# Two buffers for a batch's attention rows, and its sums of squares moved into the units of the next batch

## What is computed

```python
# 1. gated linear attention: B,H,S,D = 4, 8, 768, 48
for t in range(S):
    state = alpha[:, :, t, :, None] * state + np.einsum('bhd,bhe->bhde', k[:, :, t], v[:, :, t])
    y[:, :, t] = np.einsum('bhd,bhde->bhe', q[:, :, t], state)
x = attn_out.transpose(0, 2, 1, 3).reshape(B * S, H * D)      # 3072 rows of 384
# 2. mixture of 8 experts, one for each row, 384 -> 1024 -> 384
xn = x / (np.linalg.norm(x, axis=-1, keepdims=True) + 1e-06)  # needs a sum of squares of each row
logits = xn @ en.T / tau;  expert_idx = np.argmax(logits, axis=1)
out[mask] = gate_w[mask, None] * (np.maximum(x[mask] @ w1[e], 0.0) @ w2[e])
# 3. h = max(x @ w1, x @ w2, x @ w3), then h @ w_out, 384 -> 768 -> 384
```

## Time and profile before

| | |
|---|---|
| median of 3 runs | 801.3 us (801.27, 801.3, 805.0) |
| the profiled execution, its own time | 803.54 us |
| its span, first to last instruction | 801.8 us |
| TensorE busy (matmuls) | 749.3 us, 93% of the span |
| VectorE, GpSimd, ScalarE busy | 378.7, 296.7, 274.1 us |
| mean granted TensorE clock | 0.975 of full |

### The profile page before, as it was taken

How to read it: one execution, slowest core, us unless ns; L and a number is a source line. 1 busy time by engine, 2 the same in 40 slices (tenths; PEclk the granted TensorE clock), 3 DMA queues, 4 the chain that set the end, 5 groups by cost and what they waited for, 6 DMA issues and landing times.

```text
span 801.8 us, 15838 instructions
## 1 busy us (share of the span) xinstructions
PE 749.3 (93%) x4774; PEld 659.5 (82%) x4775; DVE 378.7 (47%) x708; ACT 274.1 (34%) x638; POOL 296.7 (37%) x226
## 2 busy tenths in 40 slices
PE   3998989989299999999999999999999999999995
PEld 3887878878269999999999888888888888888885
DVE  6787877856763343424243327533333333333321
ACT  6677776774322232222222222211211111111110
POOL 3243334410146457536275498513123131220011
PEclk9999999989689999999999999999999999999999
DMA  9966475530648154443333202101101011000001
GB/s 182 272 121 153 91 169 107 100 89 2 220 164 330 38 190 146 165 141 108 128 108 118 90 22 61 31 20 40 30 30 41 20 39 30 20 20 0 11 20 49
DMA packets 128789, 74.48 MB, mean 93 GB/s; under 512 B 103448, under 2 KB 122016, under 8 KB 128736
## 3 DMA queue, kind: packets, MB, share of 16 engines
q1 hardware_dynamic: 118624, 53.53, 24.9%
q0 software_dynamic: 4096, 10.24, 3.4%
q10 hardware_dynamic: 6016, 10.07, 3.4%
HBM read 59.03 MB, written 14.79 MB: 92 GB/s over the span
## 4 chain that ended last, share of the span: by engine, by line
PE 78%; issue 13%; DVE 3%; POOL 2%; ACT 2%; DMA 0%; ACTq 0%; POOLq 0%; DVEq 0%
PE bank L1421 55%; PE bank L1220 4%; PE bank L1313 3%; PE bank L1457 3%; PE bank L1250 3%; PE bank L1302 3%; PE bank L1281 2%; PE bank L1294 1%; PE bank L1268 1%; PE bank L1407 1%; POOL out L530 1%; DVE Sm L891 1%; PE bank L1479 1%; ACT sq L653 1%; DVE low1h L1041 1%
## 5 line engine op out<-in xcount | busy, mean ns | idle before, releaser
L490 POOL TENSOR_TENSOR wsp<-raw,wsp 128x1536 f32 x28 | 103.8, 3725 | 91.7 <-DVE wsp L1106 91.7
L1421 PE MATMUL bank<-yh,mh 128*128 128x512 f32 x324 | 128.1, 396 | 0.0
L1421 PE MATMUL bank<-yh,ml 128*128 128x512 f32 x324 | 126.5, 390 | 0.0
L530 POOL DMA_INDIRECT out<-oo,tok_t x24 | 24.2, 1010 | 199.9 <-DVE oo L1163 199.9
L1421 PE MATMUL bank<-yl,mh 128*128 128x512 f32 x324 | 91.4, 390 | 0.0
L1421 PE MATMUL bank<-wsp,xh 128*128 (+1 forms) x324 | 85.3, 398 | 3.8 <-issue 3.2
L1421 PE MATMUL bank<-wsp,hTh 128*128 x432 | 81.8, 340 | 0.0
L809 ACT CAST gh<-t 128x512 fp32r<-128x512 f32 x36 | 22.3, 620 | 151.5 <-DVE t L1174 151.5
L1421 PEld LDWEIGHTS bank<-wsp,hTh 128*128 128x128 f32 x432 | 73.9, 188 | 0.2 <-issue 0.2
L1421 PEld LDWEIGHTS bank<-wsp,xh 128*128 128x128 f32 x324 | 58.9, 188 | 15.9 <-issue 4.1
L1421 PEld LDWEIGHTS bank<-yl,mh 128*128 128x128 f32 x324 | 60.8, 188 | 13.0
(11 more groups left out here) (205 smaller groups left out, 1321.2 us busy)
## 6 DMA issues: line engine op xcount, KB each, us to landing
raw<-in_moe_w SPq DMA_DIRECT2D x16, 1536.0 KB, 7.8
expert_rows<-ye ACTq DMA_DIRECT2D x27, 193.0 KB, 3.5
yg<-expert_rows SPq DMA_DIRECT2D x24, 193.0 KB, 2.5
nat<-in_alpha SPq DMA_DIRECT2D x32, 144.0 KB, 2.7
nat<-in_k SPq DMA_DIRECT2D x32, 144.0 KB, 2.9
nat<-in_q SPq DMA_DIRECT2D x32, 144.0 KB, 3.0
vt<-in_v SPq DMA_DIRECT2D x32, 144.0 KB, 3.0
attention_rows<-xc SPq DMA_DIRECT2D x4, 1152.0 KB, 5.1
```

The source lines that it names most:

```text
L490: g.tensor_tensor(wsp[:, ds(to, 1), 1, n, part], raw[:, n:n + 1, part], wsp[:, ds(to, 1), 0, n, part].bitcast(f32), ALU.subtract).then_inc ...
L530: g.indirect_dma_start(out=out, out_offset=bass.IndirectOffsetOnAxis(ap=tok_t[:, i, 0:1], axis=0), in_=oo[i % 2][:], in_offset=None).then_ ...
L1421: last = mm(o, x, y, start=(n == 0), stop=(n == len(todo) - 1))
```

## The change

There are now two buffers `xc`, used in turn by the batches. `squares` does one chunk at a call. Of batch b-1's six, two stand in each of the units j = 0, 1, 2 of batch b: one behind `check_a`, ahead of `carry(u, 1)`, and one behind `stage_x`, ahead of the next unit's `stage_c`. The last batch's six still stand at the end. The wait for the store of rows now is for the one two batches earlier. The buffer `junk` is gone, which makes room for the second `xc`: `check_a` writes its unused copy into `kpT` (units 0 and 1) or into the `aT` whose scans are done, and `stage_a` has a wait more for that. ScalarE's and SyncE's loops over the batches are written out; those of PE, VectorE and GpSimd stay.

```diff
-    xc = sb("xc", [P, CH, DM])
+    xc = [sb(f"xc{i}", [P, CH, DM]) for i in range(2)]
-    junk = sb("junk", [P, S])
...
-            sp.dma_start(xv[:, ds(b, 1)], xc[:].rearrange("p (o c) n -> p o c n", o=1)).then_inc(x_out, 16)
+            sp.dma_start(xv[:, ds(b, 1)], xc[b % 2][:].rearrange("p (o c) n -> p o c n", o=1)).then_inc(x_out, 16)
...
-        with sp.Fori(0, B - 1) as b:
+        for b in range(B - 1):
...
             act.wait_ge(dve_A, CR + u - 1)
+            if u >= 4:
+                act.wait_ge(act_sumA, CR + u - 1)
...
         def check_a(u, j):
             act.wait_ge(act_sumA, CR + u)
-            a.activation(junk[:], A[j][:], ACT.Copy, accum_out=sums[:, 0, ds(u, 1)]).then_inc(act_sumA, 1)
+            left = (kpT[:].rearrange("p c n -> p (c n)") if u < 2 else aT[u % 2][:])
+            a.activation(left, A[j][:], ACT.Copy, accum_out=sums[:, 0, ds(u, 1)]).then_inc(act_sumA, 1)
...
         def stage_x(b, u, j):
-            if j == 0:
-
-                act.wait_ge(x_out, CR + 16 * b)
+            if j == 0 and b >= 2:
+
+                act.wait_ge(x_out, CR + 16 * (b - 1))
...
-        def squares(b):
+        def squares(b, c):
             act.wait_ge(act_X, CR + 8 * b + 8)
-            for c in range(CH):
-                act.wait_ge(act_ss, CR + CH * b + c)
-                a.activation(sq[:], xc[:, c, :], ACT.Square, accum_out=ss[:, ds(CH * b + c, 1)]).then_inc(act_ss, 1)
-
-        def step(b, j, base):
+            act.wait_ge(act_ss, CR + CH * b + c)
+            a.activation(sq[:], xc[b % 2][:, c, :], ACT.Square,
+                         accum_out=ss[:, CH * b + c:CH * b + c + 1]).then_inc(act_ss, 1)
+
+        def step(b, j):
             u = UPB * b + j
-            if j:
+            if u:
                 stage_c(u)
-            if base + j + 2 < NU:
+            if u + 2 < NU:
                 stage_a2(u + 2, (j + 2) % UPB)
             carry(u, j, 0)
-            if base + j + 2 < NU:
+            if u + 2 < NU:
                 check_a(u + 2, (j + 2) % UPB)
+            if b and j < CH // 2:
+                squares(b - 1, 2 * j)
             for c in range(1, CH - 1):
                 carry(u, j, c)
             stage_y(b, u, j)
-            if base + j + 3 < NU:
+            if u + 3 < NU:
                 stage_a(u + 3, (j + 3) % UPB)
             stage_x(b, u, j)
+            if b and j < CH // 2:
+                squares(b - 1, 2 * j + 1)
...
+        act.wait_ge(act_sumA, CR + 2)
         stage_c(0)
-        with act.Fori(0, B - 1) as b:
+        for b in range(B):
             for j in range(UPB):
-                step(b, j, 0)
-            stage_c(UPB * b + UPB)
-            squares(b)
-        for j in range(UPB):
-            step(B - 1, j, NU - UPB)
-        squares(B - 1)
+                step(b, j)
+        for c in range(CH):
+            squares(B - 1, c)
```

More of the change, by code:

```diff
@@ L204, in build @@
     assert cur[0] <= ff_low
-    router_const = (top - 4096) // 512 * 512
+    router_const = (top - 3072) // 512 * 512
     cur[0] = router_const
@@ L347, in _ @@
                 sp.wait_ge(s_done, CR + UPB * b + UPB)
-                sp.dma_start(xv[:, ds(b, 1)], xc[:].rearrange("p (o c) n -> p o c n", o=1)).then_inc(s_out, 16)
+                sp.dma_start(xv[:, ds(b, 1)], xc[0][:].rearrange("p (o c) n -> p o c n", o=1)).then_inc(s_out, 16)
         sp.wait_ge(r_hot, 1)
@@ L633, in stage_x @@
                 got = bank[6 + h][:, 0:HC * (P + E)].rearrange("p (c n) -> p c n", c=HC)
-                rows = xc[:, HC * h:HC * h + HC, HD * j:HD * j + HD]
-                a.copy(lgp[:, ds(CH * b + HC * h, HC), j, :], got[:, :, P:P + E])
+                rows = xc[b % 2][:, HC * h:HC * h + HC, HD * j:HD * j + HD]
+                a.copy(lgp[:, CH * b + HC * h:CH * b + HC * h + HC, j, :], got[:, :, P:P + E])
                 a.copy(rows.rearrange("p c (h d) -> p c h d", h=2),
@@ L642, in place @@
                 got = bank[2 + h][:, 0:HC * (P + E)].rearrange("p (c n) -> p c n", c=HC)
-                rows = xc[:, HC * h:HC * h + HC, HD * j:HD * j + HD]
+                rows = xc[0][:, HC * h:HC * h + HC, HD * j:HD * j + HD]
                 a.copy(lgp[:, ds(CH * b + HC * h, HC), j, :], got[:, :, P:P + E])
@@ L719, in _ @@
                             act.wait_ge(s_pl if c == 0 else s_sq, b + 1 if c == 0 else CR + CH * b + c)
-                            a.activation(sq[:], xc[:, c, :], ACT.Square,
+                            a.activation(sq[:], xc[0][:, c, :], ACT.Square,
                                          accum_out=ss[:, ds(CH * b + c, 1)]).then_inc(s_sq, 1)
```

## The result

The changed kernel took 790.06 us in the median of four runs (788.71 to 790.78), the one before 801.28 us in four runs beside it (800.96 to 805.0). The ratio is 0.9846, 95% interval 0.9823 to 0.987: faster by 1.5%, 11.2 us. The prediction was 786.8 us, range 784.8 to 791.0.

A forecast was written before the change was run, and what follows sets the result against it. TensorE was taken to set the attention stage's pace, waiting at batch ends for ScalarE's late states. -10.1 - 4.6 + 0.1 = -14.6, rounded to -14.5: 803.54 to 789.0, less 2.24 gives 786.8 us; range 784.8 to 791.0.

The forecast's parts named there:

- the three units: Attention units 4, 8 and 12 at the batch ends: 15.23, 15.35 and 15.96 us against 10.63 for an ordinary unit.
- The excess of 14.65 us: Time of units 4, 8 and 12 beyond 10.63 us each, all of it predicted to go.
- lateness: At batch ends, carried states come late because ScalarE does six squares first: 10.1 us, predicted to go.
- the clock: TensorE's granted clock drops to 0.50 after its idle time at batch ends: 4.6 us, predicted to go.
- The higher price of 0.74: Upper bound in us for one square, from the loop's spacing, which includes a wait for the square before.
- Unit 15: Unit 14's second square delays unit 15's `kpT`, with 0.45 us spare: costs 0.1 us, at most 0.3.
- the 2.24 us: Other runs' median lies this far below the profiled 803.54 us; subtracted from 789.0 to give 786.8 us.
- the first (squares show in part): Rival: first square delays the carries by at most 0.18 us in nine units, 1.6 us back, 788.4; chance 9%.
- the fourth (ScalarE the bound): Rival: both squares fall on the path in nine units, each gap lowering TensorE's clock: 811.6 us; chance 2%.
- first place: Between `check_a` and `carry(u, 1)` on ScalarE: cover of 1.10 us against a square's 0.52 to 0.74, costs nothing.
- The second (the clock stays low): Rival: low clock at batch ends has another cause or residual idle suffices; 4.6 us stay, 791.4; chance 4%.
- The third (the wait changes its name): Rival: something else at batch ends is late by 3.5 us or more each time, 797.3 or above; chance 3%.

The follow-up runs named there:

- the block: Changed kernel with all six squares of a batch in one block behind the next unit's kpT, where they stood before: 802.11 us, ratio 1.0009 to the kernel before.
- the second profile: The changed kernel run and profiled again with no edit: median 789.28 us, profiled execution 788.88 us.
- the third profile: The kernel before, profiled a third time with no edit: one run, 800.61 us.
- the kernel that keeps TensorE at work: Kernel before with three discarded products added ahead of TensorE's UA wait in units 4, 8 and 12, its loop written out: 798.07 us, ratio 0.9942.

## Why the prediction was right, and where it was off

- **What bounds the stage, and why the three units are long**: right. The beats are 10.63 us with the squares spread and 14.87, 13.37 and 14.90 us again with the block.
- **The excess of 14.65 us goes**: right in size, 14.55 us in the profile. Of its parts, lateness was taken too large and the clock too small: 10.1 and 4.6 us; with the clock held up the lateness is 9.0, so the clock had 5.65 in that execution. The sum counted the slow clock only in the eighteen instructions behind the carried states. Part of what it called lateness was slow clock already: at the first end the sixteen products from 74.09 us on took 1.58 us and at the third those from 168.25 on 1.97, against 1.31 at 121.19.
- **The eighteen squares cost nothing, at 0.52 us each**: right, 0.09 us after a read, the idle time for `V` nearly used up, no delay. The higher price of 0.74 would have been hidden too: with one more square there, 0.63 + 0.52 us, only 0.12 us leak through in every second unit.
- **Unit 15, 0.1 us, at most 0.3**: TensorE's wait is 0.28 us, and the last two units together are 0.35 us longer. The ceiling, not the value.
- **Second buffer, written-out code, added waits: nothing**: right, ratio 1.0009 (0.9991 to 1.0026) for these alone.
- **The time of the profiled execution, 789.0 us**: it was 790.78, and 788.88 in the second profile.
- **The step that failed** is the one ahead of the number: "The median of the other runs is 2.24 us lower, 801.3, so I predict 786.8 us". I took the 2.24 us as something that both kernels share. To a large part they are the removed part itself. The excess of the three units is 14.65 us in the profiled execution, of 803.54 us, but 11.8 us in the third profile, of 800.61 us: the low clock lasts 13.6 us there in the one and 6.8 in the other. An execution that has less of it can win only less. From 801.9 us, the median over 42 runs, to 789.5 over eight it is 12.4 us, between 11.8 and 14.65. The clock's part, 5.65 us in the profiled execution, is 801.9 - 798.07 = 3.8 us between medians, by the kernel that keeps TensorE at work (5.5 us against the eleven runs beside it, more of which were of the upper group). With it, 9.0 + 3.8 - 0.1 - 0.35 = 12.4 us, which fits.
- **What is left of the miss**: 786.8 is 3.3 us below the 790.06 measured. This step is 2.2 of them. In the other 1.0 are unit 14's square, 0.35 us where 0.1 was counted, and the collision at the start of the third layer, 1.7 us in the profiled execution; how many of the timed runs have it is not known.
- **The range held in part by luck**: the time lies in its upper part, which was kept for the first two rivals, and neither of them is what filled it.
- **Rivals**: the first (squares show in part) and the fourth (ScalarE the bound) did not happen. With two squares more in each first place TensorE does wait for ScalarE, but then it is 0.6 us a unit, not the 1.6 that would decide, and the clock stays at 1.00, where the rival let each gap lower it. The second (the clock stays low) was refuted by the profile. The third (the wait changes its name) did not happen at the batch ends, where the beat is 10.63 us; a wait that I had not named came elsewhere, 1.55 us at the start of the third layer, in one of two profiles of the changed kernel.

## What to carry to other kernels

Where an engine does a block of side work at a loop's seam while the engine that sets the pace waits, look for idle time of that same engine in the ordinary iterations, one gap for each small piece; here 0.56 and 1.12 us took 0.52 each, and nothing else of the change could be told in the time. Price a wait of TensorE by what it does to the clock as well, but not from one execution: a term that differs between executions has to be taken off the median by its own median. A profile of an execution of the lower group, the third here, showed it.

## What the runs showed of the hardware

- Much the same idle time of TensorE (1.7 to 2.1 us, then 0.4 to 0.7) was followed by 1.2 GHz in most executions and in some not: at the third batch's end the mean clock is 0.58 and 0.55 of full in two profiles from 168 to 175 us, 1.00 in a third, from the same code. The times of the kernel with these gaps fall into two groups, whose middle values are 801.0 and 803.8 us. Why the low clock stays away in some executions no run here shows.
- Idle time of TensorE of 0.3 to 0.5 us for `UA` in each of seven units (two squares more in each first place) left the clock at 1.00 from 63 to 163 us.
- Squares of 128 x 384 that wait for each other are 0.74 us apart in the loop on the chip, 0.65 written out with one wait each, and 0.71 written out with two.
- VectorE's cast of 128 x 1152 took 0.95 us alone and 3.42 us beside GpSimd's split. The Trainium skill, SBUF — State Buffer, Who interferes with whom, calls the port pair that the two share "an exclusive lock", under which, for a cast in VectorE's 2-port mode, the later of two instructions waits for the whole of the other. The rows agree within 0.2 us: GpSimd's instruction runs from 484.33 to 487.32 us, the cast starts at 484.72 and ends at 488.14, which is 0.82 us behind GpSimd's end and close to the 0.95 us that it takes alone. In which mode the cast ran no row shows. Which of the two engines comes first differs between executions of one kernel, by 1.7 us in the end.
